# Attention's scores moved two units ahead, and the first turn's weights rounded earlier in each step

## The reference

```
scores = q @ k.T / sqrt(64)            # B=2, H=8, S=576, D=64
mask   = (0 <= row - col) & (row - col < 64)
attn   = softmax(where(mask, scores, -1e9))
x      = attn @ v                      # reordered to N=1152 rows of 512
p      = domain_probs / sum(domain_probs)          # 1152 x 4
x      = sum_e p[:, e] * (relu(x @ w1[e]) @ w2[e]) # 4 experts, 512 -> 1024 -> 512
h      = x @ w_in                      # 512 -> 2048
out    = (h * cos(h)) @ w_out          # 2048 -> 512
```

## Time and profile before

| | |
|---|---|
| median of 3 runs | 681.76 us (681.07 to 683.96) |
| profiled execution | 683.99 us, span 682.2 us |
| TensorE busy | 649.3 us, 95% of the span |
| VectorE, ScalarE, GpSimd busy | 319.0, 237.7, 156.2 us |
| granted TensorE clock, mean | 0.982 |
| chain that ended last | 90% on TensorE, 3% each on VectorE, ScalarE, GpSimd |

### The profile page before, as it was taken

How to read it: one execution, slowest core, us unless ns; L and a number is a source line. 1 busy time by engine, 2 the same in 40 slices (tenths; PEclk the granted TensorE clock), 3 DMA queues, 4 the chain that set the end, 5 groups by cost and what they waited for, 6 DMA issues and landing times.

```text
span 682.2 us, 10822 instructions
## 1 busy us (share of the span) xinstructions
PE 649.3 (95%) x3960; PEld 617.4 (91%) x3960; DVE 319.0 (47%) x718; ACT 237.7 (35%) x511; POOL 156.2 (23%) x100
## 2 busy tenths in 40 slices
PE   5867789999999999999999999999999999899998
PEld 4757679999999999999999999999899999799996
DVE  4542264232423232423232423234866688866664
ACT  5752352113211113311123211126455466544453
POOL 6632210005500015400015303055600025300000
PEclk9987899999999999999999999999999999899999
DMA  9961130003400003300004200003200003001011
GB/s 286 302 222 49 62 135 1 1 1 104 144 0 1 0 0 124 123 0 0 0 10 138 99 1 0 0 32 123 93 2 0 1 32 92 1 1 47 0 46 47
DMA packets 21684, 39.59 MB, mean 58 GB/s; under 512 B 2064, under 2 KB 13328, under 8 KB 21648
## 3 DMA queue, kind: packets, MB, share of 16 engines
q1 hardware_dynamic: 21564, 39.08, 17.6%
q10 hardware_dynamic: 84, 0.02, 0.0%
HBM read 36.72 MB, written 2.38 MB: 57 GB/s over the span
## 4 chain that ended last, share of the span: by engine, by line
PE 90%; DVE 3%; ACT 3%; POOL 3%; issue 2%; POOLq 0%; ACTq 0%; DVEq 0%
PE bank L721 43%; PE bank L749 29%; PE bank L752 14%; POOL w_lo L314 2%; PE bank L713 2%; PE bank L700 1%; ACT w_hi L418 1%; ACT arena L394 1%; DVE hp_lo L550 0%; PE bank L685 0%; POOL mask L291 0%; DVE arena L583 0%; DVE arena L588 0%; DVE arena L525 0%; DVE arena L577 0%
## 5 line engine op out<-in xcount | busy, mean ns | idle before, releaser
L721 PE MATMUL bank<-x_hi,w_hi 128*128 128x384 f32 (+1 forms) x576 | 197.7, 343 | 11.6 <-POOL w_lo L314 11.3
L721 PE MATMUL bank<-x_hi,w_lo 128*128 128x384 f32 (+1 forms) x576 | 195.3, 339 | 0.0
L721 PE MATMUL bank<-x_lo,w_hi 128*128 128x384 f32 (+1 forms) x576 | 195.1, 339 | 0.0
L314 POOL TENSOR_TENSOR w_lo<-w_raw,w_hi 128x1024 fp32r<-128x1024 f32 (+1 forms) x52 | 117.4, 2261 | 331.0 <-ACT w_hi L418 325.3
L423 ACT ACTIVATE hp_hi<-h_raw 128x384 fp32r<-128x384 f32 x144 | 75.0, 523 | 304.3 <-DVE h_raw L556 282.8
L556 DVE SCALAR_TENSOR_TENSOR h_raw<-bank,p_bc 128x384 f32<-128x384 f32 x96 | 53.3, 557 | 179.7 <-PE bank L721 178.7
L749 PE MATMUL bank<-hp_hi,w_hi 128*128 128x384 f32 x384 | 130.8, 341 | 1.8 <-DVE hp_lo L550 1.8
L749 PE MATMUL bank<-hp_lo,w_hi 128*128 128x384 f32 x384 | 128.9, 336 | 0.0
L749 PE MATMUL bank<-hp_hi,w_lo 128*128 128x384 f32 x384 | 128.8, 335 | 0.0
L721 PEld LDWEIGHTS bank<-x_hi,w_hi 128*128 128x128 f32 x576 | 109.9, 191 | 15.8 <-POOL w_lo L314 12.3
L550 DVE TENSOR_TENSOR hp_lo<-h_raw,hp_hi 128x384 fp32r<-128x384 f32 x144 | 91.1, 635 | 69.6 <-ACT hp_hi L423 69.6
(11 more groups left out here) (46 smaller groups left out, 468.4 us busy)
## 6 DMA issues: line engine op xcount, KB each, us to landing
w_raw<-in_weights SPq DMA_DIRECT2D x44, 512.0 KB, 3.5
arena<-in_q SPq DMA_DIRECT2D x12, 192.0 KB, 4.8
p_bc<-p_scratch SPq DMA_DIRECT2D x4, 576.0 KB, 6.7
result<-arena SPq DMA_DIRECT2D x9, 256.0 KB, 2.1
w_raw<-in_weights SPq DMA_DIRECT2D x8, 256.0 KB, 5.6
arena<-in_k SPq DMA_DIRECT2D x8, 224.0 KB, 4.6
arena<-in_v SPq DMA_DIRECT2D x4, 384.0 KB, 3.6
arena<-in_v SPq DMA_DIRECT2D x4, 320.0 KB, 6.6
```

The source lines that it names most:

```text
L314: return nc.gpsimd.tensor_tensor(w_lo[:, f, cols], w_raw[:, f % STAGE, cols], w_hi[:, f, cols], ALU.subtract)
L721: last = nc.tensor.matmul(ps[:, 0:TOK], w[:, f, chunk(c)], x[:, c, token_cols(t)], start=c == 0 and i == 0, stop=c == DC - 1 and i == 2)
```

## The change

- **Scores two units ahead.** scores(0) and scores(1) stand ahead of the loop, and pass m has transpose(m,0), scores(m+2), transpose(m,1), outputs(m) with the up cells of x cell m-1 between them; the loop has four passes instead of five. In step f come scores(f+6). s_sb has four slots (SR). In the first four units VectorE copies the second half as well (`copy_second_early`). ScalarE takes exponentials(m+2, h) around x_high(m).
- **Weights of the first turn.** Chunk 4 is loaded ahead into the memory of h_raw (`w_ahead`), and chunks 5, 6, 7 into slots 0, 1, 2 of w_raw. ScalarE rounds chunk 5+f at the start of step f, chunk 4 in pass 2; second halves 0, 1 in passes 1, 3, second halves 2, 3 in steps 1, 2. They have semaphores of their own, for which the slots and the down cells wait.
- **Loads in order of need.** q, k of unit 1 ahead of v(0), and so on; p_bc for the first expert in two pieces, its later pieces between the loads of the units.
- **Masks.** The kinds are put in another order, so that selections cover two kinds at once. The memset and the activation of half_pi move from the start to later (ScalarE's behind the first turn).

```diff
-BOTH, SECOND, NONE_FIRST = 0, 1, 2
+NONE_FIRST, BOTH, SECOND = 0, 1, 2
@@ SyncE
+            def load_later(f):
+                slot = f - FIRST - 1
+                sp.wait_ge(second_lo_done, slot + 1)
+                sp.dma_start(w_raw[:, slot, :], weights[0, f]).then_inc(w_in_done[slot], 16)
...
+            load_qk(4)
+            load_half(0, 1, second_in)
+            load_v(3)
+            sp.dma_start(w_ahead, weights[0, FIRST]).then_inc(ahead_in, 16)
             sp.wait_ge(dp_stored, 16)
+            sp.dma_start(p_bc[:, 0, 0:TOK], ...).then_inc(p_first_tile_in, 16)
+            load_qk(5)
+            load_half(1, 1, second_in)
+            load_v(4)
+            load_half(2, 1, second_in)
+            load_later(5)
+            load_half(3, 1, second_in)
+            load_qk(6)
+            load_v(5)
+            load_later(6)
+            load_v(6)
+            load_qk(7)
+            load_later(7)
+            sp.dma_start(p_bc[:, 0, TOK:N], ...).then_inc(p_first_in, 16)
+            load_v(7)
             for e in range(1, E):
+                load_qk(7 + e)
                 sp.dma_start(p_bc[:, e, :], ...).then_inc(p_in, 16)
+                load_v(7 + e)
@@ GpSimd
+            first_block(0, slice(NONE_FIRST, NONE_FIRST + 1), 1)
+            later_block(0, slice(BOTH, SECOND + 1), 2)
+            later_block(1, slice(NONE_FIRST, BOTH + 1), 4)
+            first_block(1, slice(SECOND, SECOND + 1), 6)
...
             normalise(2, 1)
+            low_second(0)
             normalise(3, 0)
             normalise(3, 1)
             normalise(4, 0)
+            low_ahead(FIRST, w_ahead)
             normalise(4, 1)
+            for i in range(UNITS - AHEAD):
+                if i + 1 < FIRST:
+                    low_second(i + 1)
+                    low_ahead(FIRST + 1 + i, w_raw[:, i, :])
+                if AHEAD + 1 + i < UNITS:
+                    normalise(AHEAD + 1 + i, 0)
+                    normalise(AHEAD + 1 + i, 1)
@@ ScalarE
+            for m in range(AHEAD):
+                exponentials(m + 2, 0)
+                x_high(m)
+                exponentials(m + 2, 1)
+                if m == 0:
+                    high_half(2)
+                    high_half(3)
+                elif m == 1:
+                    high_second(0)
+                elif m == 2:
+                    high_ahead(FIRST, w_ahead, ahead_in)
+                else:
+                    high_second(1)
             for f in range(FC):
                 m = AHEAD + f
+                if f == 0:
+                    hidden_high(0, 0)
+                    hidden_high(1, 1)
+                    hidden_high(2, 2)
+                    hidden_high(3, 3)
+                if f < FIRST - 1:
+                    high_ahead(FIRST + 1 + f, w_raw[:, f, :], w_in_done[f])
+                    if f > 0:
+                        high_second(f + 1)
+                if m + 2 < UNITS:
+                    exponentials(m + 2, 0)
                 copy_second(m)
                 if f != FIRST:
                     hidden_high(s % FC, s)
+                if m + 2 < UNITS:
+                    exponentials(m + 2, 1)
                 x_high(m)
@@ VectorE
+            for m in range(AHEAD):
+                copy_first(m)
+                invert_sums(m + 1, 0)
+                masked_maxima(m + 2, 0)
+                copy_second_early(m)
+                invert_sums(m + 1, 1)
+                masked_maxima(m + 2, 1)
+                x_low(m)
...
+                    dve.wait_ge(p_first_tile_in, 16)
+                    dve.wait_ge(w_lo_done, FIRST + 1)
                     weigh(0, 0, 0, 0, y_ps[0])
@@ TensorE
+            scores(0)
+            scores(1)
+            pe.wait_ge(ident_done, 2)
+            for m in range(AHEAD):
+                transpose_probs(m, 0)
+                scores(m + 2)
+                if m > 0:
+                    pe.wait_ge(x_lo_done, m)
+                    up_ahead(m - 1, (0,))
+                transpose_probs(m, 1)
+                if m > 0:
+                    up_ahead(m - 1, (1, 2))
+                outputs(m)
+                if m > 0:
+                    up_ahead(m - 1, (3,))
```

More of the change, by code:

```diff
@@ L50 @@
 PR = 4
+SR = 4
 AHEAD = PAIRS
@@ L126, in build @@
         v_w = part(SLOTS, QT, P)
-        s_sb = part(2, CT, P)
+        s_sb = part(SR, CT, P)
         prob = part(PR, CT, P)
@@ L141, in build @@
         s_ps, pt_ps = bank[1:3], bank[3]
+        w_ahead = h_raw[:, :, :].rearrange("p a b -> p (a b)")[:, 0:2 * DM]
         def o_bank(m):
@@ L393, in exponentials @@
                 for t in range(CT):
-                    last = nc.scalar.activation(prob[:, g % PR, t, :], s_sb[:, g % 2, t, :], ACT.Exp,
+                    last = nc.scalar.activation(prob[:, g % PR, t, :], s_sb[:, g % SR, t, :], ACT.Exp,
                                                 bias=neg_max[:, g % PR, t:t + 1], scale=-1.0,
@@ L407, in x_high, with high_half, high_second, high_ahead @@
                 nc.scalar.activation(x_hi[x_cell(m)], o_bank(m)[:, 0:TOK], ACT.Copy).then_inc(x_hi_done, 1)
[L409 to L412, removed]
+            def high_half(f):
+                act.wait_ge(half_in[f], 16)
+                nc.scalar.activation(w_hi[:, f, 0:DM], w_raw[:, f, 0:DM], ACT.Copy).then_inc(half_hi_done, 1)
+            def high_second(f):
+                act.wait_ge(second_in[f], 16)
+                nc.scalar.activation(w_hi[:, f, DM:2 * DM], w_raw[:, f, DM:2 * DM],
+                                     ACT.Copy).then_inc(second_hi_done, 1)
+            def high_ahead(f, raw, landed):
+                act.wait_ge(landed, 16)
+                nc.scalar.activation(w_hi[:, f, :], raw, ACT.Copy).then_inc(w_hi_done, 1)
             def high_weights(f, e):
                 act.wait_ge(w_in_done[f % STAGE], w_count(e, f))
-                if not (isinstance(e, int) and e == 0):
-                    act.wait_ge(down_done, (e - 1) * TURN + (NTOK - 1) * FC + f + 1 + C_DOWN)
+                act.wait_ge(down_done, (e - 1) * TURN + (NTOK - 1) * FC + f + 1 + C_DOWN)
                 nc.scalar.activation(w_hi[:, f, :], w_raw[:, f % STAGE, :], ACT.Copy).then_inc(w_hi_done, 1)
@@ L615, in _ @@
             shares()
-            dve.wait_ge(masks, 8)
-            for m in range(AHEAD + 1):
-                if m == AHEAD:
-                    dve.wait_ge(masks, 11)
-                masked_maxima(m, 0)
-                masked_maxima(m, 1)
-                if m > 0:
-                    copy_first(m - 1)
-                invert_sums(m, 0)
-                invert_sums(m, 1)
-                if m > 0:
-                    x_low(m - 1)
+            dve.wait_ge(masks, 7)
+            masked_maxima(0, 0)
@@ L641, in _ @@
                     weigh(3, 3, 0, 0, y_ps[3])
-                if m + 1 < UNITS:
                     invert_sums(m + 1, 0)
-                if f == 0:
-                    for s in range(FIRST):
-                        hidden_low(s, s)
-                if f != FIRST:
+                    invert_sums(m + 1, 1)
+                    hidden_low(2, 2)
+                    hidden_low(3, 3)
+                    masked_maxima(m + 2, 1)
+                else:
+                    if m + 1 < UNITS:
+                        invert_sums(m + 1, 0)
+                        invert_sums(m + 1, 1)
+                    if m + 2 < UNITS:
+                        masked_maxima(m + 2, 0)
+                        masked_maxima(m + 2, 1)
+                    copy_first(m)
```

212 lines of the change are left out of this document (99 added, 113 removed).

## The result

The changed kernel took 675.04 us (median of 4 runs, 673.52 to 677.79) against 682.62 for the kernel before in the same session: a ratio of 0.9893 (95% interval 0.9861 to 0.9926), so 7.3 us or 1.1% faster by the ratio and 7.6 by the medians. Forecast were 664.2 us and 17.6 us gained, in a range from 656.5 to 673; the sign is right, the size is out by more than a factor of two. The profiled execution has a span of 674.1 us.

The account below looks back on a forecast made before the run. TensorE, stalled by late-rounded weights and slow clock in f=0 to f=3, was the bound. The stage would end at 53.3 + 13.9 + 1.6 + 6.4 + 6.9 + 12.0 = 94.1 against 111.8 us: 17.7 gained, 664.2 us, range 656.5 to 673.

Parts of the forecast that it names:

- The bound and the weights: Steps f=0 to f=3: 23.8 of 52.3 us are stalls, slow clock and gaps; all three 3.6 us weight waits go.
- The two margins of 2 us: Low halves of chunks 5 and 6: done at 41.7 and 48.7 us, needed at 43.9 and 50.8.
- The walk to the start of f=1: First units and f=0: f=0 starts at 32.4 us, f=1 at 43.0; outputs in f=0 wait 1.8 us for copy_second.
- The table's 0.7 us: ScalarE's table load at the first exponential, 6.5 us: delays the first unit by 0 to 1.28 us, 0.7 taken.
- The drain that the prediction took: ScalarE: some 1.38 us added to a table load; by it the start would be 2.7 us late.
- The load of unit 8: SP's queue: q, k of unit 8 land at 53.3 us behind chunk 7; TensorE stalls 3.4 us before f=2.
- 1.9 + 5.0: Landing of unit 8's q, k: 1.9 us fixed plus 5.0 us for 1.67 MB at 334 GB/s, from 46.4 us.
- f=2, f=3: 2 x 6.93: Steps f=2 and f=3: each takes 6.93 us, the length of the step at 91.95 us before; 13.9 together.
- f=4: 6.4: Step f=4: 6.4 us against 7.43 before, with the maxima of unit 10 ahead of copy_first on VectorE.
- f=1 by my walk has none: Steps f=0 to f=3: ScalarE's copies could make a wait in each; the walk found none in f=1.
- The 1.6 us for it: TensorE's slow clock behind the stall before f=2: between 0 and 3.6 us, 1.6 taken.
- Rival (d): TensorE kept at 1.2 GHz by many short waits from f=0 on: 43 us more, 707 us; chance 0.05.

Follow-up runs that it names:

- experiment 4: Kernel before with only the rounding moved to the start of each step and low_weights ahead of the normalisings: 667.96 us, ratio 0.9765.
- experiment 2: Changed kernel with the rest of expert 0's p_bc piece behind q, k of unit 8 and the later pieces behind units 9 and 10: 672.17 us.
- experiment 3: Changed kernel with x_high ahead of hidden_high and exponentials(m+2,1) on ScalarE, and x_low ahead of hidden_low on VectorE: 674.15 us.
- experiment 5: Changed kernel with q, k of units 8 to 10 loaded ahead of chunk 7, and x_high, x_low and copy_first moved ahead: 666.91 us.
- experiment 8: Changed kernel with q, k of units 8 to 10 loaded first, x_high, x_low and copy_first moved ahead, and no 1e-9 addition: 663.84 us.
- experiment 12: Changed kernel with q, k of units 8 to 10 first, x_high, x_low, copy_first ahead, no 1e-9 addition, copy_second ahead of exponentials(m+2,0): 657.31 us.
- experiment 9: Changed kernel with only the addition of 1e-9 to the row sums left out: 673.95 us, ratio 0.9866.
- experiment 6: Changed kernel with q, k of units 8 to 10 loaded ahead of chunk 7 and copy_first ahead of inversions and maxima: 681.02 us.
- experiment 1: Changed kernel with the loads of q, k of units 8, 9 and 10 issued before SyncE waits to load chunk 7: 669.62 us.

## Why the prediction was wrong

- **The bound and the weights: right.** The waits for w_lo were an order; alone they are worth 14.7 us (experiment 4), and in the changed kernel none is left. The two margins of 2 us held.
- **The walk to the start of f=1: right in size.** 31.7 and 42.2 against 32.4 and 43.0. The outputs in f=0 did wait for copy_second, 1.5 us against 1.8. The table's 0.7 us were not spent: its load ran at 1.5 us, ahead of the wait (the lower bound). The Trainium skill (ScalarE: Activation LUTs, Step-by-step: what each stage is for) says that the compiler places the load right before the activation; read as a time that would have been 6.5 us, and this trace disagrees: the load ran 5.0 us ahead of it, on the other side of a semaphore wait. The drain that the prediction took from the same page is not in the trace either: the second load, for the sine, runs from 463.71 for 1.28 us, and its activation starts at 465.01.
- **The load of unit 8: right in mechanism, the term too small.** The stall was named and put behind load_later(7). The landing came at 57.2 and not at 53.3, the stall was 6.1 and not 3.4 us. That is 4.0 us of the 11.0 by which the end of the stage (105.1) missed the 94.1 of the sum. Of the 4.0, 3.0 are the term "1.9 + 5.0", which measured 9.9: it had all 1.67 MB at 334 GB/s, while the p_bc piece, costed at 1.2 us, took 1.8 to 3.4 (experiment 2), and without the piece the way still took 6.6 us where the same reckoning gives 5.7. Another 0.9 is the release: chunk 7 was issued at 47.3 and not at 46.4, since ScalarE came to chunk 6 at 44.4 and not at 43.3, behind the same x_high as in the next item.
- **The steps behind it: the step that failed.** "f=2, f=3: 2 x 6.93" and "f=4: 6.4" took a step's length from the steps of before in which nothing waits. The prediction costed the work of each engine and walked ScalarE's list in f=0 and f=1, but it left out a wait of that list: hidden_high(f+4) writes the slot that down(f) reads, and so waits for the end of the step. Before, x_high stood right behind it; now exponentials(m+2,1) stand between, 1.25 us, and x_high comes so much later. On VectorE copy_first now has two inversions and six maxima ahead of it behind x_low. The waits name both, and experiment 3 shows the second growing when the first is gone. They were not all: with both out of the way (experiment 5) the steps took 8.2 us, and 6.93 came only when the additions and the place of copy_second behind three exponentials were gone too (experiments 8 and 12). The walk had found the wait for copy_second in f=0 and written "f=1 by my walk has none"; behind the two other waits it did not show in the changed kernel's later steps. In f=2 and f=3 together it was 17.9 us against 15.5 (the slow clock included), in f=4 11.2 against 6.4: 7.2 us in all, and f=5 to f=7 were as forecast (18.8 against 18.9). 4.0 + 7.2 is the miss. In f=2 all of it is the slow clock behind the load's stall (TensorE was busy 8.99 of 8.99 us); in f=3 and f=4 it is these waits and the clock behind them.
- **The wait for GpSimd: not seen.** The 193 ns of the earlier trace rows was a mean over instances of about 0.16 us with one of 0.84 in it, at 17.93 us, behind a GpSimd subtraction; a look at the longest would have shown it. In the changed kernel it cost about 1 to 2 us (experiment 9), but it decided 12 us in experiment 6.
- **The clock.** The 1.6 us for it were 2.1 in f=2, behind the stall, and f=4's two waits (2.1 and 1.8 us) brought another fall, a granted clock of 0.70. Rival (d) had too long a reach: in experiment 1, with two gaps of 0.8 us in each of f=1 to f=3, the clock stayed at 1.00 there.
- **The range.** It left room for one late chunk, but none for steps whose length was copied and not walked; its upper side was 8.8 us (673 less 664.2), and those steps' 7.2 with the load's 4.0 are 11.2.

## What to carry to other kernels

When a wait is taken away, walk every engine's list for at least one more step than the one that was bound, with each semaphore that its instructions wait for, above all those that free a slot; a step's length copied from an undisturbed stretch holds only for the order of that stretch. A transfer that is needed soon should not stand in a queue behind one that must wait for a slot, nor, as far as experiment 2 shows, behind a broadcast to all partitions. Undo or apply the parts one by one: here one part alone gave twice the gain of the whole, and the whole gave its worth only after four more orders were set right and an addition was left out. Compare the steps that an edit touches and not only the times of the whole kernel: a difference of one to three microseconds can come from another place.

## What the runs showed of the hardware

In these traces a VectorE TENSOR_SCALAR from SBUF to SBUF waits until the GpSimd TENSOR_TENSOR that runs has ended. The changed kernel has five such instances (1.16, 0.45, 1.03, 0.24 and 1.77 us), and each ends within 0.05 us of a GpSimd piece; the other 19 take 0.14 to 0.17. The longest (timeline, GpSimd and VectorE):

```profile
28.31 2.38 POOL L343 TENSOR_TENSOR w_lo<-h_raw,w_hi 128x1024 fp32r<-128x1024 f32 x1
...
28.94 1.77 DVE L588 TENSOR_SCALAR arena<-arena 128x3 f32<-128x3 f32 x1
...
30.75 0.17 DVE L590 RECIPROCAL arena<-arena 128x3 f32<-128x3 f32 x1
```

1.77 us for three columns (0.16 when GpSimd idles), ending at 30.7 with the subtraction. The RECIPROCAL over the same columns does not: without the addition it took 0.17 us in the midst of a subtraction, in experiment 9:

```profile
29.48 2.38 POOL L343 TENSOR_TENSOR w_lo<-h_raw,w_hi 128x1024 fp32r<-128x1024 f32 x1
...
30.19 0.17 DVE L588 RECIPROCAL arena<-arena 128x3 f32<-128x3 f32 x1
```

The Trainium skill (SBUF — State Buffer, SBUF: two separate sides) says that VectorE in a mode with two ports and GpSimd lock a pair of ports for a whole instruction and the other waits; the trace agrees in the wait, with the 1.77 us here and the 12.4 us of the 24 additions in experiment 6. That this addition runs in such a mode, no run here shows.

While the broadcast of one p_bc row over 128 partitions was among the transfers, the queues moved 232 GB/s at a share of 1.01, and 340 at 1.03 in the 5 us behind it; that later stretch had a broadcast in it too, so what sets the rate stays open.

The granted clock does not fall behind every wait of the same length. Some 95 us before the end, in the last layer, TensorE waits 2.8 us for VectorE to take outputs out of a bank (L634), in every kernel alike. In some executions the clock falls behind this wait, in others not; five microseconds around that place in experiment 8 and in the changed kernel:

```profile
562.90:567.90 5.00, 3.15 (x7) 2.49 (x8) 5.00 (x7) 2.98 (x5) 2.36 (x2) 0.59 0.01 3
574.00:579.00 5.00, 2.16 (x13) 1.80 (x12) 4.93 (x6) 2.08 (x4) 2.47 (x2) 1.00 0.00 0
```

From the scores of f=5 to the end it makes 591.2 us in the one and 587.7 in the other, while the program there is the same. What decides it, no run here shows; the 1.4 us in "the rest" between the kernels before and after, and 3.5 us between experiments 8 and 12, are of this kind.
